# First MLP of a fused attention + MoE kernel: another order of the Mish factors, a clamp on GpSimd, and the second product four steps behind

## What is computed

```
h = x @ w_in                      # 1536 x 512 by 512 x 2048
sp = where(h > 20, h, log1p(exp(min(h, 20))))
g = h * tanh(sp)                  # Mish
x2 = g @ w_out                    # 1536 x 2048 by 2048 x 512
```

## Time and profile before

| | |
|---|---|
| median of 3 runs | 998.47 us (997.83 to 1001.27) |
| span of the profiled execution | 997.3 us |
| PE busy | 901.0 us (90%) |
| DVE busy | 531.2 us (53%) |
| ACT busy | 320.7 us (32%) |
| POOL busy | 274.9 us (28%) |
| mean granted TensorE clock | 0.964 |

### The profile page before, as it was taken

One profiled execution on the slowest core, in us unless ns is written; L12 is line 12 of the kernel. 1 busy time (PEld: TensorE's weight loads), 2 busy tenths in 40 slices (PEclk: granted clock), 3 DMA queues, 4 the chain that ended last, 5 costly groups with the idle time before them and its releaser, 6 DMA issues.

```text
span 997.3 us, 13387 instructions
## 1 busy us (share of the span) xinstructions
PE 901.0 (90%) x4880; PEld 464.9 (47%) x4880; DVE 531.2 (53%) x1005; ACT 320.7 (32%) x689; POOL 274.9 (28%) x225
## 2 busy tenths in 40 slices
PE   3776997779996998779989999999999999999998
PEld 2665886624442443334334444444444444444443
DVE  6685769789759975969765131341213413122121
ACT  3565897635426452534340110101101001010010
POOL 1194900872212221213100930019300193000000
PEclk9797999889998999789999999999999999999999
DMA  9711160031000000000220040000400000001001
GB/s 187 236 34 32 36 198 1 4 124 46 1 0 0 0 0 1 0 1 1 85 84 1 0 168 0 1 0 0 168 1 1 0 0 0 0 4 39 21 21 42
DMA packets 49979, 38.32 MB, mean 38 GB/s; under 512 B 39696, under 2 KB 39696, under 8 KB 49424
## 3 DMA queue, kind: packets, MB, share of 16 engines
q1 hardware_dynamic: 49936, 37.78, 12.8%
HBM read 34.63 MB, written 3.15 MB: 38 GB/s over the span
## 4 chain that ended last, share of the span: by engine, by line
PE 71%; DVE 11%; issue 8%; POOL 5%; ACT 4%; DMA 1%; SPq 0%; DVEq 0%; ACTq 0%; POOLq 0%
PE bank L494 57%; PE bank L518 9%; DVE wpieces L830 2%; PE bank L413 2%; POOL wB L583 2%; ACT tmp L683 1%; PE bank L450 1%; PE bank L431 1%; POOL stage L578 1%; POOL wB L580 1%; DVE tmp L1056 1%; DVE hid L1050 1%; PE bank L391 1%; ACT tmp L704 1%; DVE tmp L1046 1%
## 5 line engine op out<-in xcount | busy, mean ns | idle before, releaser
L494 PE MATMUL bank<-xT,wA 128*128 (+1 forms) x1152 | 265.5, 389 | 36.2 <-DVE tmp L1056 30.9
L494 PEld LDWEIGHTS bank<-xT,wA 128*128 128x128 f16 x1152 | 114.6, 100 | 180.8 <-DVE tmp L1056 34.2
L764 ACT ACTIVATE hid<-bank 128x512 f16<-128x512 f32 x96 | 57.4, 598 | 409.6 <-PE bank L494 409.6
L1117 DVE SCALAR_TENSOR_TENSOR hid<-bank,hid 128x512 f16<-128x512 f32 x96 | 66.3, 690 | 158.7 <-ACT hid L764 158.6
L518 PE MATMUL bank<-hid,wB 128*128 128x512 f16 x576 | 130.2, 379 | 2.4 <-DVE hid L1050 2.4
L494 PE MATMUL bank<-xT,wB 128*128 x576 | 125.3, 379 | 0.0
L494 PE MATMUL bank<-wB,hid 128*128 128x512 f16 x576 | 125.3, 379 | 0.0
L494 PE MATMUL bank<-wA,hid 128*128 128x512 f16 x576 | 125.3, 379 | 0.0
L627 POOL TENSOR_TENSOR tmp<-tmp 128x512 f32<-128x512 f32 x48 | 66.6, 1388 | 172.7 <-DVE tmp L1065 165.4
L1132 DVE SCALAR_TENSOR_TENSOR acc<-bank,pg,acc 128x512 f32 (+1 forms) x36 | 27.0, 751 | 137.1 <-PE bank L494 137.1
L518 PEld LDWEIGHTS bank<-hid,wB 128*128 128x128 f16 x576 | 56.0, 98 | 71.1 <-DVE hid L1050 4.1
(11 more groups left out here) (99 smaller groups left out, 956.5 us busy)
## 6 DMA issues: line engine op xcount, KB each, us to landing
stage<-in_moe_w SPq DMA_DIRECT2D x8, 2048.0 KB, 8.9
stage<-in_moe_w_in SPq DMA_DIRECT2D x1, 4096.0 KB, 14.2
stage<-in_moe_w_out SPq DMA_DIRECT2D x1, 4096.0 KB, 13.8
hid<-in_q SPq DMA_DIRECT2D x16, 192.0 KB, 3.7
hid<-in_k SPq DMA_DIRECT2D x16, 192.0 KB, 4.1
xT<-in_v SPq DMA_DIRECT2D x8, 384.0 KB, 6.4
out_y<-acc SPq DMA_DIRECT2D x12, 256.0 KB, 2.0
pr<-in_moe_domain_probs SPq DMA_DIRECT2D x1, 24.0 KB, 13.8
```

The source lines that it names most:

```text
L494: last = pe.matmul(dst, lhs(c, a), rhs(c, b), start=(c == 0 and n == 0), stop=(c == chunks - 1 and n == 2))
L764: act.activation(hv[:, f, 0, :], psum(f % 4), ACT.Relu).then_inc(h_hi, 1)
L1117: dve.scalar_tensor_tensor(hv[:, f, 1, :], psum(f % 4), 0.0, hv[:, f, 0, :], ALU.max, ALU.subtract).then_inc(h_ready, 1)
```

## The change

The factors are multiplied in another order: h is taken into the product first (b = -h n, straight from PSUM, when n is there), and the corrected reciprocal last, on POOL. The clamp of u moves from DVE to POOL. `r_t` has two buffers instead of three and `g_t` three instead of two. LAG is 4. ACT and DVE do the high and low part for step j - 2 instead of j - 3.

```diff
-        u_t, n_t, r_t, g_t = temps[0:2], temps[2:5], temps[5:8], temps[8:10]
+        u_t, n_t, r_t, g_t = temps[0:2], temps[2:5], temps[5:7], temps[7:10]
-        LAG = 5
+        LAG = 4
@@ PE
-                            pe.wait_ge(g_ready, FT * g + step - 3)
+                            pe.wait_ge(b_ready, FT * g + step - 3)
@@ POOL
-                for f in range(FT):
-
-                    pool.wait_ge(q_ready, FT * g + f + 1)
-                    pool.tensor_tensor(n_t[f % 3], n_t[f % 3], r_t[f % 3], ALU.mult).then_inc(t_ready, 1)
-                    if isinstance(g, int) and g == NG - 1 and f == 6:
+                for f in range(FT + 1):
+                    if f < FT:
+
+                        pool.wait_ge(u_ready, FT * g + f + 1)
+                        pool.sem_inc(carrier, 1)
+                        pool.tensor_scalar(u_t[f % 2], u_t[f % 2], U_MAX, None, ALU.min).then_inc(um_ready, 1)
+                    if f > 0:
+                        m = f - 1
+                        pool.wait_ge(q_ready, FT * g + m + 1)
+                        pool.tensor_tensor(g_t[m % 3], g_t[m % 3], r_t[m % 2], ALU.mult).then_inc(g_ready, 1)
+                    if isinstance(g, int) and g == NG - 1 and f == PIECES:
@@ ACT
+                        if j >= 2:
+                            act.wait_ge(n_ready, FT * g + j - 1)
                         act.activation(u_t[j % 2], psum(j % 4), ACT.Exp, scale=inv_h).then_inc(u_ready, 1)
@@ ACT, step m = j - 1
-                        act.activation(r_t[m % 3], n_t[m % 3], ACT.Ln, bias=two).then_inc(l_ready, 1)
+                        if m >= 2:
+                            act.wait_ge(g_ready, FT * g + m - 1)
+                        act.activation(r_t[m % 2], n_t[m % 3], ACT.Ln, bias=two).then_inc(l_ready, 1)
@@ ACT
-                    if 0 <= j - 3 < FT:
-                        m = j - 3
+                    if 0 <= j - 2 < FT:
+                        m = j - 2
                         act.wait_ge(g_ready, FT * g + m + 1)
-                        act.activation(hv[:, m, 0, :], g_t[m % 2], ACT.Copy).then_inc(h_hi, 1)
+                        act.activation(hv[:, m, 0, :], g_t[m % 3], ACT.Copy).then_inc(h_hi, 1)
@@ DVE
-                        dve.wait_ge(u_ready, FT * g + j + 1)
-                        dve.tensor_scalar(u, u, U_MAX, None, ALU.min).then_inc(n_step, 1)
-                        dve.wait_ge(n_step, FT * g + j + 1)
+                        dve.wait_ge(um_ready, FT * g + j + 1)
                         dve.scalar_tensor_tensor(n, u, 2.0, u, ALU.add, ALU.mult).then_inc(n_ready, 1)
-                    if 0 <= j - 3 < FT:
-                        m = j - 3
-                        dve.wait_ge(h_hi, FT * g + m + 1)
-                        dve.tensor_tensor(hv[:, m, 1, :], g_t[m % 2], hv[:, m, 0, :], ALU.subtract).then_inc(h_ready, 1)
+                        if j >= 3:
+                            dve.wait_ge(h_ready, FT * g + j - 2)
+                        dve.wait_ge(n_ready, FT * g + j + 1)
+                        dve.scalar_tensor_tensor(g_t[j % 3], psum(j % 4), -1.0, n,
+                                                 ALU.mult, ALU.mult).then_inc(b_ready, 1)
                     if 0 <= j - 2 < FT:
                         m = j - 2
-                        dve.wait_ge(t_ready, FT * g + m + 1)
-                        if m >= 2:
-                            dve.wait_ge(h_ready, FT * g + m - 1)
-                        dve.scalar_tensor_tensor(g_t[m % 2], psum(m % 4), -1.0, n_t[m % 3],
-                                                 ALU.mult, ALU.mult).then_inc(g_ready, 1)
+                        dve.wait_ge(h_hi, FT * g + m + 1)
+                        dve.tensor_tensor(hv[:, m, 1, :], g_t[m % 3], hv[:, m, 0, :], ALU.subtract).then_inc(h_ready, 1)
```

More of the change, by code:

```diff
@@ L246, in program @@
         x2_step = sem("x2_step")
-        u_ready, n_step, n_ready = sem("u_ready"), sem("n_step"), sem("n_ready")
-        l_ready, r_ready, t_ready = sem("l_ready"), sem("r_ready"), sem("t_ready")
+        u_ready, um_ready, n_ready, b_ready = sem("u_ready"), sem("um_ready"), sem("n_ready"), sem("b_ready")
+        l_ready, r_ready = sem("l_ready"), sem("r_ready")
         e_ready, q_ready = sem("e_ready"), sem("q_ready")
@@ L735, in first_mlp @@
                         act.wait_ge(n_ready, FT * g + m + 1)
-                        act.activation(r_t[m % 3], n_t[m % 3], ACT.Ln, bias=two).then_inc(l_ready, 1)
+                        if m >= 2:
+                            act.wait_ge(g_ready, FT * g + m - 1)
+                        act.activation(r_t[m % 2], n_t[m % 3], ACT.Ln, bias=two).then_inc(l_ready, 1)
                         act.wait_ge(l_ready, FT * g + m + 1)
-                        act.activation(r_t[m % 3], r_t[m % 3], ACT.Exp, scale=-1.0).then_inc(r_ready, 1)
-                    if 0 <= j - 3 < FT:
-                        m = j - 3
+                        act.activation(r_t[m % 2], r_t[m % 2], ACT.Exp, scale=-1.0).then_inc(r_ready, 1)
+                    if 0 <= j - 2 < FT:
+                        m = j - 2
                         act.wait_ge(g_ready, FT * g + m + 1)
-                        act.activation(hv[:, m, 0, :], g_t[m % 2], ACT.Copy).then_inc(h_hi, 1)
+                        act.activation(hv[:, m, 0, :], g_t[m % 3], ACT.Copy).then_inc(h_hi, 1)
                     if isinstance(g, int) and g == NG - 1 and j >= FT - 1:
@@ L1042, in first_mlp @@
                         u, n = u_t[j % 2], n_t[j % 3]
-                        dve.wait_ge(u_ready, FT * g + j + 1)
-                        dve.tensor_scalar(u, u, U_MAX, None, ALU.min).then_inc(n_step, 1)
-                        dve.wait_ge(n_step, FT * g + j + 1)
+                        dve.wait_ge(um_ready, FT * g + j + 1)
                         dve.scalar_tensor_tensor(n, u, 2.0, u, ALU.add, ALU.mult).then_inc(n_ready, 1)
-                    if 0 <= j - 3 < FT:
-                        m = j - 3
-                        dve.wait_ge(h_hi, FT * g + m + 1)
-                        dve.tensor_tensor(hv[:, m, 1, :], g_t[m % 2], hv[:, m, 0, :], ALU.subtract).then_inc(h_ready, 1)
+                        if j >= 3:
[3 more added lines that the diff above has]
+                                                 ALU.mult, ALU.mult).then_inc(b_ready, 1)
                     if 0 <= j - 2 < FT:
                         m = j - 2
-                        dve.wait_ge(t_ready, FT * g + m + 1)
-                        if m >= 2:
-                            dve.wait_ge(h_ready, FT * g + m - 1)
-                        dve.scalar_tensor_tensor(g_t[m % 2], psum(m % 4), -1.0, n_t[m % 3],
-                                                 ALU.mult, ALU.mult).then_inc(g_ready, 1)
+                        dve.wait_ge(h_hi, FT * g + m + 1)
+                        dve.tensor_tensor(hv[:, m, 1, :], g_t[m % 3], hv[:, m, 0, :], ALU.subtract).then_inc(h_ready, 1)
                     if 0 <= j - 1 < FT:
                         m = j - 1
-                        n, r = n_t[m % 3], r_t[m % 3]
+                        n, r = n_t[m % 3], r_t[m % 2]
                         dve.wait_ge(r_ready, FT * g + m + 1)
```

## The result

| | before | after |
|---|---|---|
| median | 998.4 us | 1091.3 us |
| span of the profiled execution | 997.3 us | 1087.2 us |
| ratio after / before | | 1.092, 95% interval 1.090 to 1.094 |

The forecast was 1048 us, 1036 to 1060. The direction and the way were right and the size was not: 93 us were lost where 49 were forecast.

A forecast was written before the change was run, and what follows sets the result against it. PE bound the kernel before; the new POOL-DVE loop would make Mish the bound. Losses of 12.0, 16.5 and 20.9 us in groups 0, 1 and 2 sum to 49.4, giving 1048 us, range 1036 to 1060.

The forecast's parts named there:

- The serial loop between POOL and DVE: In every Mish step POOL and DVE work one after the other, 5.50 us a step against PE's 5.18.
- The price of the clamp: POOL's clamp on 128x512 float32 in each step, taken as 0.68 us.
- the bound of 0.90: Upper bound for POOL's clamp, from the 768-column TENSOR_SCALAR row as it stands: 0.90 us.
- 38 turns: Clamp-to-clamp turns of POOL and DVE counted over the groups, each put at 5.50 us.
- the three T: Start of each group's first clamp: 212.9 us in group 0, then 18.2 and 18.4 us after the previous group's end.
- the opening of group 2: Line 830 on DVE delays the third clamp once, to 7.34 us after the first instead of 6.21.
- the clamp costs as much as the product: Rival: POOL's clamp takes 1.27 us and the loop 6.09, for a total time of 1073 us; chance 0.04.
- The head start lost in group 0: DVE's n(0) to n(2) no longer overlap POOL's w_out split; group 0 ends 12.0 us later.
- The switch behind the carrier: Groups 1 and 2: POOL's 7.0 us config after the reduction waits for u; group 1 ends 16.5 us later.
- The switch in the middle of group 2 counts in full: POOL's switches around its reductions delay clamp(9) to 59.3 us after the first clamp instead of 45.8.
- LAG 4 costs nothing by itself: PE's second product waits for a low part whose needed first product PE has already done; no cost.
- The faster rival: Loop stays under PE's 5.18 us step and the switch stays hidden: 6.6 us less, 992 us; chance 0.07.

The follow-up runs named there:

- experiment 4: Changed kernel with POOL's order turned, clamp(j+1) before product(j-1), same instructions and engines: 1035.7 us, ratio 1.036.
- experiment 3: Changed kernel with the clamp of u back on DVE, all else as changed (LAG 4): 1005.1 us, ratio 1.005.
- Experiment 1: Changed kernel with POOL's clamp replaced by a multiplication by 1.0 twice, so no clamping: 1046.2 us, ratio 1.047.
- experiment 5: Changed kernel with one tiny ordinary POOL operation at the head of each group, ahead of the carrier: 1083.9 us, ratio 1.086.
- experiment 6: Changed kernel with LAG 5 instead of 4: 1090.5 us, ratio 1.092.
- experiment 7: Kernel before with LAG 4 instead of 5 and nothing else: 1003.9 us, ratio 1.005.
- experiment 9: Changed kernel with clamp and product both on DVE, POOL out of Mish, reordered factors kept, LAG 5: 970.6 us, ratio 0.972.
- experiment 11: Kernel before, its order of factors kept, with only POOL's product moved to DVE: 979.3 us, ratio 0.979.
- experiments 8: Changed kernel with the clamp back on DVE and LAG 5: 1001.7 us, ratio 1.003.

## Why the prediction was wrong

- *The serial loop between POOL and DVE*: right. The waits of the changed kernel show it in every step, experiment 4 (order alone, 56 us back) and experiment 3 (clamp away, 86 us back) confirm it.
- *The price of the clamp*: this term was wrong, and it makes nearly all of the miss. It was scaled from rows of TENSOR_SCALAR with multiplications, and the bound of 0.90 was taken from the same rows. min takes 1.48 us. 0.80 us more in 48 clamps is 38 us, and with n to b at 0.79, 0.07 more in 38 turns, 41. Against that stand 1.6 us by which the three T came sooner in sum, and 0.8 in the opening of group 2, which grew by one clamp and not by two: that leaves 38.7 of the 38.5 by which the groups' sum missed (87.9 less 49.4). Experiment 1 gives the multiplication's price and 1046 us. The range had a second fault: it moved the clamp in 38 turns only, and left out the ten others, so that even a clamp of 0.90 was put 2 us too cheap. The rival "the clamp costs as much as the product" (1.27 us, 1073) stood on the right side with a chance of 0.04 and was still too cheap. That no row showed a min on POOL had been said; the bound was too narrow all the same.
- *The head start lost in group 0*: right in kind. T came at 210.3 instead of 212.9.
- *The switch behind the carrier*: right, shown by its start at 326.8 and by experiment 5 (7.5 us against 8.2).
- *The switch in the middle of group 2 counts in full*: product(7) ends at 510.4 and the next clamp starts at 523.84, 13.4 us, as forecast, and PE waited up to 14.4 us.
- *LAG 4 costs nothing by itself*: true for this kernel (experiment 6), wrong as a general statement: 5 us in the kernel before (experiment 7).
- *The faster rival* needed a turn below 5.18 us and an early switch. Experiments 9 and 11 show that the idea behind it, the reordered factors with the early release, is worth 9 us once nothing on POOL stands in Mish.

What stays open: why min costs so much on POOL (only its price was measured), and how experiments 3 and 8 split their missed gain between the stretched n, POOL's split in group 0 and the reduction in group 2; the run with POOL out removes all three at once. That the gain of experiment 11 comes from the switches is read from where it lies; no run kept POOL's product and dropped only the switches.

## What to carry to other kernels

When two engines serve each other in one step, write down the order in which each takes its instructions and follow the ring until it comes back: if clamp, product and their partner's work all lie on it, their lengths add, and an engine that is 30% busy can bind the kernel. An operation's price on an engine is that of its arithmetic, not only of its shape: bound an unseen one by the dearest that the engine shows, and wider. A stage that never catches up hands every late start on to its end, so look first whether it has slack, and try the version with the slow helper left out: here it gave 970.6 us, 2.8% below the kernel before.

## What the runs showed of the hardware

- On GpSimd a 128x512 float32 tensor_scalar took 0.62 us with two multiplications, 1.48 with a min, 1.92 with a min and a multiplication. The same min took 0.42 us on DVE.
- GpSimd's switch from partition_all_reduce back to ordinary operations took 6.8 to 7.8 us from config to operation (517.0 to 523.8 in the changed kernel, 323.4 to 331.2 in experiment 5), and waited behind a semaphore increment that itself waited. With no ordinary operation between two reductions it cost nothing: in experiment 9 the config stands at 373.8 and the reduction at 373.96.
- Moving an operation of 1.27 us from GpSimd to DVE, where it takes 0.69, made DVE's step shorter (4.73 to 4.52 us, experiments 8 and 9), since an operation of DVE that had been stretched by 0.95 us beside it no longer was.
- After TensorE had stood still for 7.25 us its granted clock was 0.50 from 217.2 to 221.2 us, and 24 matmuls took 7.69 us instead of 5.35 (kernel before).
